# Last first-chunk outputs issued in two rounds; the range check of w spread over Pool and ScalarE

## The reference, cut to what matters

```
for t in range(S):
    cur = einsum('bhd,bhe->bhde', u * k_t, v_t)
    y_t = einsum('bhd,bhde->bhe', r_t, state + cur)
    state = w * state + einsum('bhd,bhe->bhde', k_t, v_t)
x = y as [B*S, H*D]                      # 3072 x 384
x = ((x @ w_a) * (x @ w_b)) @ w_out      # 384 -> 1536 -> 384
h = x @ w_in;  g = h * clip(h + 3, 0, 6) / 6
out = g @ w_out2                         # 384 -> 2048 -> 384
```

## Time and profile before

| | us |
|---|---|
| median of 3 runs | 919.6 (919.18 to 920.41) |
| the profiled execution, device time | 919.12 |
| its span, first to last instruction | 917.3 |
| busy: TensorE | 911.9 (99%) |
| busy: VectorE, ScalarE, Pool | 369.5, 329.5, 184.3 |

### The profile page before, as it was taken

One profiled execution on the slowest core, in us unless ns is written; L12 is line 12 of the kernel. 1 busy time (PEld: TensorE's weight loads), 2 busy tenths in 40 slices (PEclk: granted clock), 3 DMA queues, 4 the chain that ended last, 5 costly groups with the idle time before them and its releaser, 6 DMA issues.

```text
span 917.3 us, 15108 instructions
## 1 busy us (share of the span) xinstructions
PE 911.9 (99%) x6400; PEld 746.4 (81%) x6400; DVE 369.5 (40%) x607; ACT 329.5 (36%) x651; POOL 184.3 (20%) x168
## 2 busy tenths in 40 slices
PE   8999999999999999999999999999999999999998
PEld 6788888888888888888888888888888888888887
DVE  7746344525443343334222343343343343343332
ACT  6645323232333233242221343433333333333333
POOL 5976102111111111010755570000000000000000
PEclk9999999999999999999999999999999999999999
DMA  8653211121120121131311210100200100100000
GB/s 307 198 167 108 90 50 62 55 90 56 56 110 34 56 110 55 38 129 48 115 50 55 78 50 1 65 5 1 69 1 0 70 1 7 64 0 1 35 1 36
DMA packets 24281, 57.84 MB, mean 63 GB/s; under 512 B 2320, under 2 KB 8080, under 8 KB 24208
## 3 DMA queue, kind: packets, MB, share of 16 engines
q1 hardware_dynamic: 19808, 48.18, 15.6%
q10 hardware_dynamic: 4400, 8.65, 2.5%
HBM read 47.39 MB, written 9.44 MB: 62 GB/s over the span
## 4 chain that ended last, share of the span: by engine, by line
PE 98%; DVE 1%; DMA 0%; ACT 0%; issue 0%; SPq 0%; DVEq 0%; ACTq 0%
PE up_ps L722 32%; PE up_ps L799 21%; PE acc_ps L736 16%; PE acc_ps L813 11%; PE att_ps L813 11%; PE att_ps L614 2%; PE att_ps L677 1%; PE att_ps L682 1%; PE att_ps L646 1%; PE att_ps L663 1%; PE att_ps L671 1%; DMA first_rk<-in_rk_turned 0%; ACT A L854 0%; DVE first_rk L1044 0%; DVE first_A L1067 0%
## 5 line engine op out<-in xcount | busy, mean ns | idle before, releaser
L722 PE MATMUL up_ps<-x_cut,w_up 128*128 128x512 f32 x1296 | 307.3, 391 | 0.2 <-ACT x_cut L867 0.2
L722 PEld LDWEIGHTS up_ps<-x_cut,w_up 128*128 128x128 f32 x1296 | 241.7, 188 | 52.9 <-issue 3.0
L926 ACT ACTIVATE g_cut<-tmp 128x512 fp32r<-128x512 f32 x168 | 106.2, 632 | 214.4 <-DVE tmp L1149 141.6
L1157 DVE SCALAR_TENSOR_TENSOR g_cut<-tmp,g_cut 128x512 fp32r<-128x512 f32 x168 | 125.2, 745 | 117.5 <-ACT g_cut L926 117.5
L736 PE MATMUL acc_ps<-g_cut,w_down 128*128 128x512 f32 x648 | 157.3, 390 | 0.0
L736 PEld LDWEIGHTS acc_ps<-g_cut,w_down 128*128 128x128 f32 x648 | 121.3, 188 | 26.0 <-issue 0.6
L1151 DVE SCALAR_TENSOR_TENSOR tmp<-tmp,up_ps 128x512 f32<-128x512 f32 x96 | 66.1, 689 | 182.9 <-ACT tmp L920 182.9
L920 ACT ACTIVATE tmp<-up_ps,three 128x512 f32<-128x512 f32 x96 | 66.2, 690 | 171.0 <-PE up_ps L799 171.0
L1149 DVE TENSOR_TENSOR tmp<-tmp,up_ps 128x512 f32<-128x512 f32 x72 | 49.5, 688 | 169.7 <-PE up_ps L722 169.6
L799 PE MATMUL up_ps<-x_cut,w_up 128*128 128x512 f32 x432 | 105.7, 389 | 0.0
L799 PE MATMUL up_ps<-x_cut,w_in_first 128*128 128x512 f32 x432 | 105.4, 389 | 0.0
(11 more groups left out here) (109 smaller groups left out, 557.2 us busy)
## 6 DMA issues: line engine op xcount, KB each, us to landing
nat<-in_natural SPq DMA_DIRECT2D x20, 704.0 KB, 6.0
rkT<-in_rk_turned SPq DMA_DIRECT2D x20, 512.0 KB, 3.6
w_raw<-in_moe_w_out SPq DMA_DIRECT2D x28, 192.0 KB, 2.4
layer_out_T<-stage ACTq DMA_DIRECT2D x6, 768.0 KB, 3.4
x_cut<-layer_out_T SPq DMA_DIRECT2D x6, 768.0 KB, 4.3
outT<-stage ACTq DMA_DIRECT2D x5, 768.0 KB, 3.3
w_raw<-in_moe_w_in SPq DMA_DIRECT2D x12, 256.0 KB, 4.6
first_rk<-in_rk_turned SPq DMA_DIRECT2D x4, 512.0 KB, 5.6
```

The costliest lines, as they stand in the source:

```text
L722: mm = pe.matmul(up_ps[:, m, :], w_up[i // PB][:, a, m, c, cols], x_cut[:, t % 2, b, c, :], start=(z == 0), stop=(z == len(order) - 1))
L926: nc.scalar.activation(g_cut[:, n % GR, HI, :], tmp[:, n % 2, :], ACT.Copy, scale=1.0 if n < TILES * N1 else 1.0 / 6.0).then_inc(s_gh, 1)
L1157: dve.scalar_tensor_tensor(out=lo, in0=tmp[:, n % 2, :], scalar=1.0 if n < TILES * N1 else 1.0 / 6.0, in1=hi.bitcast(F32), op0=ALU.mult, o ...
```

## The change

It has four parts.

1. For chunk 3 alone, `outputs` runs in two rounds: the late steps (64 to 127) as soon as the first of the three masks is done, the early steps (0 to 63) after all three. The number of matmul instructions for that chunk doubles, each with half the columns.
2. The two comparisons of w move from VectorE to Pool, as three operations (two comparisons and a product), put after the fourth of Pool's eight mask operations. TensorE's count waits for the third of them.
3. The flag is made by one ScalarE activation, Relu(count + 1 - 3·W2·NP) written as an integer, in the place of two VectorE operations. Pool sets the bias by one more memset. The count stands in another PSUM bank.
4. w and u are loaded through ScalarE's queue, as its first instruction, and not through SyncE's. One product of zeros (`keep_warm(pe, 2)`) after the count is gone.

```
@@ first_loads
-            sp.dma_start(w_u_col[0:W2], w_u_pairs).then_inc(s_w_u, 16)
             load_first_rk(sp, 0)
@@ new, called in make_masks after the fourth keep_where
+        def find_in_range(pool):
+            pool.wait_ge(s_w_u, 16)
+            nc.gpsimd.tensor_scalar(in_range[0:W2], w_col[0:W2], W_MIN, None, ALU.is_ge).then_inc(s_guard, 1)
+            nc.gpsimd.tensor_scalar(not_above[0:W2], w_col[0:W2], W_MAX, None, ALU.is_le).then_inc(s_guard, 1)
+            pool.wait_ge(s_guard, 2)
+            nc.gpsimd.tensor_tensor(out=in_range[0:W2], in0=in_range[0:W2], in1=not_above[0:W2],
+                                    op=ALU.mult).then_inc(s_guard, 1)
@@ outputs
-            pe.wait_ge(s_A, MASKS * (q + 1))
-            (main and rest matmuls over all steps)
+            for steps, masks_done in (((slice(MID, CH), 1), (slice(0, MID), MASKS)) if q == B - 1 else
+                                      ((slice(0, CH), MASKS),)):
+                pe.wait_ge(s_A, MASKS * q + masks_done)
+                (main and rest matmuls over those steps)
@@ guard_and_tables, now tables_of_powers
-            dve.tensor_scalar(in_range[0:W2], w_col[0:W2], W_MIN, None, ALU.is_ge).then_inc(s_guard, 1)
-            dve.wait_ge(s_guard, 1)
-            dve.scalar_tensor_tensor(out=in_range[0:W2], in0=w_col[0:W2], scalar=W_MAX, in1=in_range[0:W2],
-                                     op0=ALU.is_le, op1=ALU.mult).then_inc(s_guard, 1)
             (four scans)
-            dve.wait_ge(s_count, 1)
-            dve.tensor_scalar(all_in[:], count_ps, 3.0 * W2 * NP - 1.0, None, ALU.is_ge).then_inc(s_guard, 1)
-            dve.wait_ge(s_guard, 3)
-            dve.tensor_copy(flag[:], all_in[:]).then_inc(s_flag, 1)
@@ scalar
+                act.dma_start(w_u_col[0:W2], w_u_pairs).then_inc(s_w_u, 16)
-                act.wait_ge(s_three, 1)
+                act.wait_ge(s_three, 2)
                 nc.scalar.activation(first_use[:], three[:], ACT.Copy)
+                act.wait_ge(s_count, 1)
+                nc.scalar.activation(flag[:], count_ps, ACT.Relu, bias=all_but_one[:, 0:1]).then_inc(s_flag, 1)
                 flag_act = decide(act)
@@ tensor
-                pe.wait_ge(s_guard, 2)
+                pe.wait_ge(s_guard, 3)
                 (four matmuls of the count)
                 keep_warm(pe, 4)
-                keep_warm(pe, 2)
                 first_chunks(pe)
```

More of the change, by code:

```diff
@@ L109, in build @@
             in_range = sb("in_range", [P, NP], of=setup)
-            all_in = sb("all_in", [1, 1], of=setup)
+            not_above = sb("not_above", [P, NP], of=setup)
+            all_but_one = sb("all_but_one", [1, 1], of=setup)
             inv_fine = sb("inv_fine", [P, NP, FINE + 1], of=setup)
@@ L306, in x_view @@
             return x_cut[:, tile % 2, z, :, cols_of(q)]
-        count_ps = acc_ps[0:1, 1, 0:1]
+        count_ps = att_ps[0:1, 0, 0:1]
         HD = H * D
@@ L497, in make_masks @@
             keep_where(P + MID, every, 1, -1, 0, 1, ALU.is_equal)
+            find_in_range(pool)
             keep_where(2 * P, low_half, 1, -1, 0, 1, ALU.is_gt)
@@ L672, in outputs @@
                               start=True, stop=False, skip_group_check=True)
-            pe.wait_ge(s_A, MASKS * (q + 1))
[L674 to L683, removed]
+            for steps, masks_done in (((slice(MID, CH), 1), (slice(0, MID), MASKS)) if q == B - 1 else
+                                      ((slice(0, CH), MASKS),)):
+                pe.wait_ge(s_A, MASKS * q + masks_done)
+                for half in range(2):
+                    for p in range(NP):
+                        part = slice(EM * p, EM * (p + 1))
+                        pe.matmul(main[half][part, steps], v_nat(q)[:, 2 * p + half, 0:EM], A_at(q, half)[:, p, steps],
+                                  start=(not earlier and half == 0 and steps.stop == CH), stop=True,
+                                  skip_group_check=True)
+                for half in range(2):
+                    for p in range(NP):
+                        part = slice(EM * p, EM * (p + 1))
+                        mm = pe.matmul(rest[part, steps], v_rest(q)[:, 2 * p + half, :], A_at(q, half)[:, p, steps],
+                                       start=False, stop=(half == 1), skip_group_check=True)
             mm.then_inc(s_y, 1)
@@ L1182, in vector_layer2, with tables_of_powers @@
                         x2_low(dve, t + 1)
-        def guard_and_tables(dve):
+        def tables_of_powers(dve):
             links = [0]
@@ L1268, in _ @@
                 nc.gpsimd.memset(three[:], 3.0).then_inc(s_three, 1)
+                nc.gpsimd.memset(all_but_one[:], 1.0 - 3.0 * W2 * NP).then_inc(s_three, 1)
                 make_masks(pool)
@@ L1301, in _ @@
             def _(dve):
-                guard_and_tables(dve)
+                tables_of_powers(dve)
                 flag_dve = decide(dve)
```

## The result

The changed kernel takes 926.35 us (median of 6, 925.85 to 926.99) against 919.69 before (919.18 to 920.41): a ratio of 1.0073, interval 1.006 to 1.0086. The prediction was 918.8 with a range to 920.3.

What follows compares the result with a forecast made beforehand. TensorE's solid matmul stream from 20.55 us was taken as the bound, so only its start could move. The head's 0.35 plus the rounds' 0.44 gave 0.79 won, 919.6 - 0.8 = 918.8 us, range 918.0 to 920.3.

Steps and rivals of the forecast that it cites:

- What bounds the kernel, and the start as the only place: TensorE streams matmuls from 20.55 us to the end; time won ahead of that start is won on the whole.
- Part 4: Load of w on ScalarE's queue: r and k land 0.45 us earlier; sharing the DMA delays w by zero, at most 2.25.
- the near row: Overlap of a ScalarE store with SyncE's weight loads at 449 us: loads land in 2.3 against 2.4, so contention costs nothing.
- The 0.45 on the issue of r and k: Without w's issue ahead on SyncE, loads of r and k start at 0.80 us and not 1.25.
- my 4.75: Forecast landing of r and k of chunk 0, in us, 0.45 earlier than before.
- Parts 2 and 3: Comparisons on Pool win VectorE 0.29 us, flag on ScalarE 0.10; together 0.38 to 0.39, Pool's operations taking 0.6 to 0.8.
- 0.1 to 0.2 covers this: TensorE's slack in us, before chunk 0's product ends, said to absorb the later count from Pool's slower comparisons.
- The dropped filler: Product of zeros behind the count: TensorE stays as busy in total up to 5.3 us without it.
- Part 1: Chunk 3's outputs: only the second round stays behind the last mask, 0.67 us against 1.11, so 0.44 won.
- Late w: Rival at the start: w lands late behind r and k; full 2.25 us late gives 921.0; chance 0.28.
- the clock: Rival on TensorE: rise to 2.4 GHz after chunk 0's own weights loses 0.9 us, 919.7, up to 920.7; chance 0.08.
- a chance of 0.04: Chance of a slower verdict for the whole kernel: w at its upper bound, or the clock with it.

Runs made afterwards that it cites:

- run 9: Kernel before with comparisons on Pool, flag on ScalarE, and two of its ten zero blocks moved ahead of TensorE's wait for the comparisons: 919.10 us, 0.9997.
- run 8: Kernel before with only the comparisons on Pool and the flag on ScalarE; w on SyncE, filler kept, one round of outputs: 921.19 us, 1.0022.
- Run 6: Kernel before with one edit, the two-block product of zeros behind the count taken away: 921.26 us, 1.0024.
- run 4: Kernel before with the two rounds of chunk 3's outputs alone: 923.57 us, 1.0051.
- runs 3: Changed kernel with one more 512-column product of zeros ahead of TensorE's wait for the comparisons: 925.41 us, 1.007.
- 16: Kernel before with r and k of chunk 0 loaded through ScalarE's queue, w still first on SyncE's: 921.27 us, 1.0024.
- Run 12: Kernel before with 12 tiny products of zeros, 48 records, put into TensorE's wait ahead of chunk 3's outputs: 921.66 us, 1.0027.
- run 13: Changed kernel, all parts kept, with six more blocks of zeros ahead of TensorE's wait for the comparisons: 923.79 us, 1.0041.
- run 10: Kernel before with w and u on ScalarE's queue and one more product of zeros ahead of TensorE's wait for the comparisons: 921.9 us, 1.0026.
- run 7: Changed kernel with w back on SyncE's queue and chunk 3's outputs in one round; filler still dropped: 924.12 us, 1.0053.
- 11: Kernel before with chunk 3's outputs in two rounds for only the first 32 columns of each head: 919.6 us, 1.0.
- run 15: Changed kernel with w on SyncE, two zero blocks ahead of the wait and none dropped, two rounds for the first 32 columns only: 919.83 us, 1.0009.
- point 14: A note, not a run: a wait for instructions seems to cost again through half clock in some executions, mean granted clock 0.998; untested.

## Why the prediction was wrong, point by point

**What bounds the kernel, and the start as the only place.** Right. From the first dense product to the last, the streams before and after run in step.

**Part 4.** This step failed first. I took zero for the contention, "the near row", and 2.25 us as the bound. It was 2.09 late (4.58 against 2.49). The row was not near: at 449 us the packets are of 1536 and 2048 bytes on the two queues, none as short as w's 48, and they overlap only in part. The 0.45 on the issue of r and k was right (0.80), and they landed even 0.35 ahead of my 4.75 (at 4.40). It was useless, since VectorE's arm was the later one.

**Parts 2 and 3.** The prices were right: Pool's three operations 0.24, 0.22 and 0.20, 0.82 with their waits (0.6 to 0.8 forecast), ScalarE's flag 0.25, and 0.39 earlier at the dense product once nothing else is wrong (run 9). What failed is "0.1 to 0.2 covers this" for TensorE. I asked only whether the pause would be on the chain. It is not, and still costs, through the clock (run 8).

**The dropped filler** I costed at nothing, with TensorE "as busy in total" as its reason. Run 6 is this edit alone: 1.9 us in the median.

**Part 1.** The price of the second round was right, 0.66 against 0.67. What failed is that a doubled number of instructions was priced in matmul time alone. Nothing in my sum stood for their supply: 1.90 us in run 4, 0.87 in the changed kernel. (The 1.44 us there are not of this part, as run 4 says. Waits of 0.6 us or more at the 450th record show in four profiles, those of the changed kernel and runs 3, 8 and 16, and in all four the clock rose near 12 or 13 us.) Run 12 shows that any 48 records do it. The trace of before had no such wait, since its 706th record lay inside the dense product, where TensorE consumes a record every 0.11 us.

**The rivals.** Late w was one of them (0.28), at its upper bound 921.0, and the clock another (0.08), 919.7 to 920.7. Both happened. I named the two together only in a chance of 0.04, without a price, and did not see that the first brings the second: the late w is what idles TensorE. The clock was mis-sized too. I let it cost the own weights of one chunk or two; it stayed down to 13 to 20 us. Its share is 2.2 to 2.6 us with all parts in place (run 13) and 4.7 with one round (run 10).

**The sum as it was.** w late: 2.4 (run 10). The clock: 2.2 to 2.6 (run 13). Parts 2 and 3 win 0.4. That leaves some 2.1 to 2.5 of the 6.7 for the rounds with their wait. The shares don't add up freely: each cause hides part of another, as run 7 shows for the rounds and run 13 for the wait.

**What stays open.** Why the packet with the 706th record comes so late: it starts at 19.3 to 21.4 in the kernel before and in runs 4, 11, 12, 13 and 15, and at 23.1 in the changed kernel, and no run shows what sets that start. How three of 11 executions in run 15 come to 921 and more was not seen in a profile; one of them, 923.71, has the granted clock of 0.998 that point 14 speaks of, the other two do not. No version beats the kernel before: run 9 is 0.4 us lower in the median, within its interval.

## What to carry to other kernels

Filler that holds TensorE's clock is part of the critical path, though it is on no chain of waits: keep it without pauses, and when a wait moves, move filler in front of it. A small load that everything waits for belongs ahead of the large ones in one queue, not beside them in another. Where TensorE runs hundreds of narrow matmuls in a row, count the instructions that an edit adds, as they have to arrive too.

## What the runs showed of the hardware

- In nine profiles TensorE had no pause over 0.13 us ahead of 4.9 us, and the clock rose at 4.5 to 7.2 us. In the other eight it had one, of 0.23 to 2.44 us at 3.2 or of 0.79 at 4.9, and the clock rose at about 12 to 20.6 us, while narrow matmuls kept the engine busy. Not every execution pays: with the pause of 0.23 (run 8), or with 256 columns of zeros less (run 6), the same program scattered by 5 to 6 us. That the low clock is the state at the start and that activity ends it is also what the Trainium skill says ("TensorE: Matmul & The Clock Gate", "Part 1: The HAM clock gate"); the trace agrees (2.08 us for a pair of zeros at the start, 1.12 later).
- The windows view gives a granted clock of 1.00 ahead of the first recorded change, though the lengths of the matmuls show half speed (2.08 against 1.12 for the same pair). At the start of a kernel, lengths are the thing to read.
- A load of 5.2 KB in rows of 48 bytes took 1.6 to 1.8 us alone, 2.8 beside rows of 4096 bytes when it was first, and 3.8 to 3.9 when it was second.
- TensorE's instructions came in packets of 16384 bytes, and the waits for them stood 256 records apart (at the 450th and the 706th). 48 records without work cost 2.2 us where they moved the 706th ahead of the dense product (run 12).
